# Low parts written over the exponents, head copies ahead of a high part, and the first chunk prepared a pair sooner, in an attention and two-MLP kernel

## The chip, the cores and the metric

The kernel runs on one core of a Trainium2 chip. The metric is the device time of one execution in microseconds (us), as the median of several runs. The engines of a core work side by side, each through its own list of instructions: TensorE (matmuls), ScalarE (ACT), VectorE (DVE), the Pool engine (GpSimd, POOL) and SyncE (SP), whose list here is nearly all DMA issues. They wait for each other by semaphores.

## What is computed

Attention over 4 x 8 heads, then two MLPs, all fp32:

```python
scores = scale * np.matmul(q, k.transpose(0, 1, 3, 2))      # 32 heads, 576 x 576, head_dim 64
thresh = np.max(scores, axis=-1, keepdims=True) - tau
scores = np.where(scores >= thresh, scores, -1000000000.0)
attn = softmax(scores)
x = (attn @ v) laid out as [2304, 512]
x = ((x @ w_a) * (x @ w_b)) @ w_out                          # d_ff 1536
h = x @ w_in                                                 # d_ff 1024
out = (layer_norm(h * softmax(h)) * g_ln) @ w_out2
```

## The kernel before

Each fp32 operand of a matmul is split into a high part, rounded by a copy into `fp32r`, and a low part, the difference of the two. A product is then three matmuls (high x high, high x low, low x high). The attention product of q and k packs parts so that two matmuls do. TensorE's list is written out by hand and so is that of every other engine.

**Pairs and slots.** The 32 heads go through in 16 pairs. A pair has 9 slots (`SLOTS`), one for each tile of 128 keys: head 0 of the pair has tiles 0 to 3 and half of tile 4, head 1 the other half of tile 4 and tiles 5 to 8. `MID` is 4. In slot s of a pair TensorE does, in this order (L1132 to L1143):
- `scores(s)` of the *next* pair, 4 matmuls (8 in slot 4), for the row maxima alone. It needs the maximum before it (`max_done`), since all use one PSUM place;
- `scores_t(s)` of this pair, 4 matmuls (8 in slot 4), the transposed scores. It needs `mask(s - 2)`, whose PSUM place it takes;
- `values`, the P·V matmuls at L1104. Head 0's first ones stand in slot 3, its last in slot 7; head 1's first ones in slot 8, its last in slot 2 of the next pair. The first ones of a head wait until the head before is copied out of PSUM (`head_out`).

A tile's way from `scores_t(s)` is: ScalarE `exps(s)` (L600) writes exponents to `prob`; VectorE `mask(s)` (L840) zeroes those under the threshold, reading PSUM and `prob`; ScalarE `high_probs(s)` (L607) makes `p_hi`; the Pool engine's `low_probs(s)` (L529) makes `p_lo = prob - p_hi`; TensorE reads both. `prob` has 3 places (`RAW`), `p_hi` and `p_lo` 6 each (`RP`). `exps` waits until the `p_lo` three tiles back is made.

In a slot ScalarE does, in order: `high_max` (slots 0 and 5), `exps(s)`, `high_probs(s - 1)`, then `high_v` (slots 0, 5) or `high_qk` (slots 1, 6). `copy_head` (L614) stands ahead of `exps` in slots 3 and 8. VectorE does the maximum of `scores(s)` (L826), `mask(s - 1)`, then `turn_max` (L834, slots 0 and 5), `low_qk` (L817, slots 2 and 7), `invert` (slot 6). The Pool engine does `low_max` (L537, slots 0 and 5), `split_v` (slots 1, 6), `low_probs(s - 1)`. `turn_max` needs `low_max`, `low_max` needs `high_max`. In an engine's list nothing overtakes.

SyncE deals the operands of the heads ahead: `deal_first` (zeros and high parts), `deal_low`, and the maxima by way of DRAM (`store_max`, `load_max`); it also moves finished heads to `xT` (`move_head`), spreads the row sums and stores their inverses.

**The first MLP** starts in the last pair. Its tokens go in 6 chunks of 384. Chunk 0 is prepared early: `load_inverse` (L387) brings the inverse row sums to `inverse_first`, `normalize` (L852) multiplies `xT` by them in 4 pieces, `high_x` (L634) and `low_x` (L864) split the pieces, `high_w` (L628) and `low_w` (L858) the first weights, which `load_w` (L454) brings. TensorE's `up(0, 0)` has 8 pieces; it does four of them in slots 5 to 8 of the last pair and the others between the last P·V parts. In the kernel before, `load_inverse` stands ahead of SyncE's list for pair 14, all four `normalize` pieces stand in slot 8 of pair 14, and the splits in slots 0 to 6 of pair 15. Pairs are counted from 0.

Of the kernel before, what the change touches and what calls it, by code (L numbers as in the profile page):

```python
# [23 lines left out]
P = 128  # L24
# [11 lines left out]
def build_program(nc, qkT, v_tiles, tau, w_a, w_b, w_o, w_in, w_out, g_col, eye, out):  # L36
# [20 lines left out]
    ROLL = 4  # L57
# [7 lines left out]
    RAW = 3  # L65
    RP = 6
    assert SLOTS % RAW == 0 and 2 * SLOTS % RP == 0
# [4 lines left out]
    with outer:  # L72
# [16 lines left out]
        with ExitStack() as a:  # L89
# [16 lines left out]
            prob = sb(a, "prob", [P, RAW, S])  # L106
            p_hi = sb(a, "p_hi", [P, RP, S], F32R)
            p_lo = sb(a, "p_lo", [P, RP, S], F32R)
# [200 lines left out]
        def _(sp):  # L309
# [91 lines left out]
            def step(i, e):  # L401
# [4 lines left out]
                head(load_max, i, e, 1)  # L406
                head(load_qk, i, e + 3, 0)
# [9 lines left out]
                head(load_max, i, e + 1, 0)  # L417
                pair(store_inverse, i, e - 1)
# [40 lines left out]

            for r in range(2):  # L460
                sp.wait_ge(inverse_out[r], 16 * (LAST_PAIR_OF_CHUNK_0 // 2 + (1 if r == 0 else 0)))
            load_inverse(0, inverse_first)
            step(last, 0)
            load_w(0)
# [35 lines left out]
        def _(pool):  # L500
# [23 lines left out]
            def low_probs(i, e, s):  # L524
# [3 lines left out]
                at_least(pool, pv_done, used_up(i, e, s, RP))  # L528
                pool.tensor_tensor(p_lo[:, r, :], prob[:, s % RAW, :], p_hi[:, r, :].bitcast(F32),  # L529
# [52 lines left out]
        def _(act):  # L582
# [13 lines left out]
            def exps(i, e, s):  # L596
                n, ps = number(i, e, s), st_ps[(SLOTS * e + s) % 2]
                act.wait_ge(st_done, n + 1)
                at_least(act, p_lo_done, n + 1 - RAW)
                act.activation(halves(prob[:, s % RAW, :]), ps[:, :, 0:HALF], ACT.Exp,  # L600
                               scale=SCALE).then_inc(exp_done, 1)

            def high_probs(i, e, s):
# [3 lines left out]
                act.activation(p_hi[:, r, :], prob[:, s % RAW, :], ACT.Copy).then_inc(p_hi_done, 1)  # L607
# [28 lines left out]
            def early(s):  # L636
                if s < NK:
                    if s == 0:
                        act.wait_ge(ops_in[ROLL - 1], dealt(last, ROLL - 1))
                    high_x(0, (s,))  # L640
                elif s < NK + 2:
                    high_w(0, (s - NK,))

            def step(i, e):
                for s in range(SLOTS):
                    ni, ne = pair_at(i, e + 1)
                    if s == 3 and not (isinstance(i, int) and 2 * i + e == 0):
                        pi, pe = pair_at(i, e - 1)
                        copy_head(pi, 2 * pe + 1)
# [4 lines left out]
                    if s == SLOTS - 1:  # L654
                        copy_head(i, 2 * e)
                    exps(i, e, s)
# [13 lines left out]
                    if isinstance(i, int) and 2 * i + e == PAIRS - 1:  # L670
                        early(s)
# [136 lines left out]
        def _(dve):  # L808
# [27 lines left out]
            def mask(i, e, s):  # L836
                n, ps = number(i, e, s), st_ps[(SLOTS * e + s) % 2]
                dve.wait_ge(exp_done, n + 1)
                p = halves(prob[:, s % RAW, :])
# [27 lines left out]
            def step(i, e):  # L867
                for s in range(SLOTS):
# [459 lines left out]
```

## Time and profile before

| | |
|---|---|
| median of 3 runs | 1017.98 us (1016.18 to 1018.18) |
| the profiled execution | 1015.74 us, its span 1013.60 us |
| TensorE busy | 975.0 us (96%) |
| VectorE, ScalarE, Pool engine busy | 536.9, 415.4, 256.3 us |
| TensorE granted clock | 1.00 |
| attention | about 0 to 345 us |

The span is the time from the first to the last instruction. TensorE is busy nearly everywhere; the Pool engine works only in the attention part, where VectorE is busy for about 79% of the time. Matmuls overlap by their pipelines: one of 288 columns is shown as 0.29 us, but the next starts 0.13 us after it.

### The profile page before, as it was taken

Reading aid. Unit: us, or ns where it says so; the run is one execution under the profiler, and the core shown is the slowest. Engines: PE = TensorE matmul, PEld = TensorE weight load, DVE = VectorE, ACT = ScalarE, POOL = GpSimd, SP = SyncE. Lnnn points to the kernel's source line nnn. Section 1 sums busy time; section 2 is a strip of 40 time slices with the busy share of each in tenths; the row PEclk is TensorE's granted clock in tenths of the full one; section 3 lists DMA queues with packets and bytes.
Section 4 is the critical chain, followed back from the end, with each engine's and each line's share of the span. In section 5 each row is a group of like instructions: output and inputs, shape, how many; then the busy total and the mean of one; then the engine's idle time right before and its main releaser. Section 6 shows DMA issues by size and latency. Waiting matters only on the chain.

```text
span 1013.6 us, 16645 instructions
## 1 busy us (share of the span) xinstructions
PE 975.0 (96%) x5844; PEld 924.3 (91%) x5844; DVE 536.9 (53%) x863; ACT 415.4 (41%) x739; POOL 256.3 (25%) x242
## 2 busy tenths in 40 slices
PE   5999999999998999999999999999999999999997
PEld 4999999999997999999999999999999878888886
DVE  7787878777877654321321321221223676655664
ACT  3677767777776644211211211211212422223321
POOL 3777777777777400000000000000000000000000
PEclk9999999999999999999999999999999999999999
DMA  7566666666663343210010010000020200000000
GB/s 184 148 157 156 147 152 156 161 148 150 150 151 85 108 144 108 62 32 1 1 31 0 0 31 0 0 0 0 0 83 1 82 21 21 21 21 23 28 21 31
DMA packets 51566, 71.31 MB, mean 70 GB/s; under 512 B 14552, under 2 KB 24920, under 8 KB 51536
## 3 DMA queue, kind: packets, MB, share of 16 engines
q1 hardware_dynamic: 51536, 70.94, 27.0%
q8 instruction: 16, 0.26, 0.1%
q14 instruction: 14, 0.11, 0.0%
HBM read 33.25 MB, written 5.32 MB: 38 GB/s over the span
## 4 chain that ended last, share of the span: by engine, by line
PE 91%; issue 4%; DMA 1%; SPq 1%; DVE 1%; ACT 1%; POOL 0%; POOLq 0%; DVEq 0%; ACTq 0%
PE PS L1104 12%; PE PS L1121 10%; PE PS L1123 10%; PE PS L1122 10%; PE PS L1067 8%; PE PS L1069 8%; PE PS L1191 5%; PE PS L1189 5%; PE PS L1190 5%; PE PS L1248 3%; PE PS L1250 3%; PE PS L1249 3%; PE PS L1224 3%; PE PS L1222 3%; PE PS L1223 3%
## 5 line engine op out<-in xcount | busy, mean ns | idle before, releaser
L529 POOL TENSOR_TENSOR p_lo<-prob,p_hi 128x576 fp32r<-128x576 f32 x144 | 210.1, 1460 | 80.4 <-ACT p_hi L607 79.2
L1067 PE MATMUL PS<-ops 128*128 128x288 f32 x642 | 179.2, 301 | 15.9 <-DVE ops L902 6.8
L1121 PE MATMUL PS<-x_hi,w_ab_rolled 128*128 128x384 f32 x576 | 192.5, 334 | 1.6 <-issue 1.6
L1123 PE MATMUL PS<-x_hi,w_ab_rolled 128*128 128x384 f32 x576 | 192.4, 334 | 0.0
L1122 PE MATMUL PS<-x_lo,w_ab_rolled 128*128 128x384 f32 x576 | 192.4, 334 | 0.0
L1069 PE MATMUL PS<-ops 128*128 128x288 f32 x642 | 176.2, 296 | 0.0
L941 DVE TENSOR_TENSOR gate<-gate,PS 128x384 f32<-128x384 f32 x72 | 39.9, 554 | 253.5 <-ACT gate L707 253.5
L707 ACT ACTIVATE gate<-PS 128x384 f32<-128x384 f32 x72 | 35.4, 492 | 268.7 <-PE PS L1123 268.7
L1067 PEld LDWEIGHTS PS<-ops 128*128 128x128 f32 x642 | 121.4, 189 | 21.0 <-issue 8.1
L826 DVE TENSOR_REDUCE neg_max<-PS 128x1 f32<-128x576 f32 x144 | 107.6, 749 | 47.4 <-PE PS L1069 46.4
L1069 PEld LDWEIGHTS PS<-ops 128*128 128x128 f32 x642 | 121.6, 189 | 0.0
L607 ACT ACTIVATE p_hi<-prob 128x576 fp32r<-128x576 f32 x144 | 98.6, 684 | 51.1 <-DVE prob L840 42.2
L840 DVE SCALAR_TENSOR_TENSOR prob<-PS,neg_tau,prob 128x576 f32<-128x576 f32 x144 | 116.2, 807 | 2.7 <-ACT prob L600 2.7
L568 POOL MEMSET halfpow<- 128x1 f32 x1 | 0.1, 104 | 448.0 <-PE PS L1191 448.0
L1121 PEld LDWEIGHTS PS<-x_hi,w_ab_rolled 128*128 128x128 f32 x576 | 108.2, 188 | 1.8 <-issue 1.8
L1122 PEld LDWEIGHTS PS<-x_lo,w_ab_rolled 128*128 128x128 f32 x576 | 108.1, 188 | 0.0
L1123 PEld LDWEIGHTS PS<-x_hi,w_ab_rolled 128*128 128x128 f32 x576 | 108.1, 188 | 0.0
L600 ACT ACTIVATE prob<-PS 128x576 f32<-128x576 f32 x144 | 92.9, 645 | 35.5 <-PE PS L1069 30.9
L1189 PE MATMUL PS<-g_hi,w_od 128*128 128x384 f32 x288 | 96.2, 334 | 0.0
L1190 PE MATMUL PS<-g_lo,w_od 128*128 128x384 f32 x288 | 96.2, 334 | 0.0
L1191 PE MATMUL PS<-g_hi,w_od 128*128 128x384 f32 x288 | 96.2, 334 | 0.0
L1104 PE MATMUL PS<-p_hi,v_hi 128*65 128x288 f32 x320 | 68.8, 296 | 13.7 <-issue 13.6
(91 smaller groups left out, 1530.5 us busy)
## 6 DMA issues: line engine op xcount, KB each, us to landing
qk_raw<-qkT_dram SPq DMA_DIRECT2D x32, 288.0 KB, 3.1
ops<-qk_hi SPq DMA_DIRECT2D x62, 144.0 KB
ops<-qk_hi SPq DMA_DIRECT2D x31, 288.0 KB
ops<-qk_lo SPq DMA_DIRECT2D x62, 144.0 KB
v_raw<-v_tiles_dram SPq DMA_DIRECT2D x32, 160.0 KB, 2.5
xT<-head_sb SPq DMA_DIRECT2D x32, 144.0 KB, 3.2
out_dram<-o_sb SPq DMA_DIRECT2D x18, 256.0 KB, 2.0
stage<-inverse_dram SPq DMA_DIRECT2D x20, 192.0 KB, 3.9
```

Source lines behind the costliest of these rows:

```text
L529: pool.tensor_tensor(p_lo[:, r, :], prob[:, s % RAW, :], p_hi[:, r, :].bitcast(F32), ALU.subtract).then_inc(p_lo_done, 1)
L826: dve.tensor_reduce(out=neg_max[:, e, s:s + 1], in_=ps[:, :, 0:HALF], axis=AX_XY, op=ALU.max, negate=True).then_inc(max_done, 1)
L840: dve.scalar_tensor_tensor(out=p, in0=ps[:, :, 0:HALF], scalar=neg_tau[:, 0:1], in1=p, op0=ALU.is_ge, op1=ALU.mult).then_inc(mask_done, 1)
L1067: pe.matmul(ps[:, b, 0:HALF], weights[0][:, r, own], moving[0][:, r, cols], start=(n == 0), stop=False)
L1069: ins = pe.matmul(ps[:, b, 0:HALF], weights[1][:, r, own], moving[1][:, r, cols], start=False, stop=(n == len(parts) - 1))
L1104: ins = pe.matmul(o_ps[0:D + 1, b, 0:HALF], v[:, side, t, :], p[:, r, b * HALF:(b + 1) * HALF], start=(t == 0 and part == 0), stop=(t == N ...
L1121: pe.matmul(bank, w[:, 0, :], x_hi[:, k, :], start=(k == 0), stop=False)
L1122: pe.matmul(bank, w[:, 0, :], x_lo[:, k, :], start=False, stop=False)
L1123: ins = pe.matmul(bank, w[:, 1, :], x_hi[:, k, :], start=False, stop=(k == NK - 1))
L1189: pe.matmul(bank, w[:, 0, :], g_hi[:, f % 2, :], start=(f == 0), stop=False)
L1190: pe.matmul(bank, w[:, 0, :], g_lo[:, f % 2, :], start=False, stop=False)
L1191: ins = pe.matmul(bank, w[:, 1, :], g_hi[:, f % 2, :], start=False, stop=(f == NF - 1))
```

## The change

- `p_lo` gets 9 places and `prob` the same 9 places in the same memory; the Pool engine writes `p_lo(s)` over `prob(s)`. `exps` waits for the P·V that last read the place, one pair back; `low_probs` waits for no P·V.
- `copy_head` moves from ahead of `exps` in slots 3 and 8 to behind `exps` in slots 2 and 7, ahead of a `high_probs`.
- SyncE issues `load_inverse` within its list for pair 14, behind the operands of head 31, and `load_w(0)` a few steps sooner.
- `normalize` goes one piece at a time into slots 5 to 8 of pair 14, `high_x` into slots 6 to 8 of pair 14 and slot 0 of pair 15, `high_w` into slots 1 and 2, `low_x` into slots 0 to 2, `low_w` into slots 3 and 4 of pair 15.
- TensorE's `up(0, 0)` starts in slot 4 of pair 15.

```diff
-    RAW = 3
...
-            prob = sb(a, "prob", [P, RAW, S])
+            with ExitStack() as same:
+                prob = sb(same, "prob", [P, SLOTS, S])
+            p_lo = sb(a, "p_lo", [P, SLOTS, S], F32R)
             p_hi = sb(a, "p_hi", [P, RP, S], F32R)
-            p_lo = sb(a, "p_lo", [P, RP, S], F32R)
...
                 head(load_max, i, e, 1)
+                if isinstance(i, int) and 2 * i + e == PAIRS - 2:
+                    for r in range(2):
+                        sp.wait_ge(inverse_out[r], 16 * (LAST_PAIR_OF_CHUNK_0 // 2 + (1 if r == 0 else 0)))
+                    load_inverse(0, inverse_first)
                 head(load_qk, i, e + 3, 0)
...
                 head(load_max, i, e + 1, 0)
+                if isinstance(i, int) and 2 * i + e == PAIRS - 2:
+                    load_w(0)
                 pair(store_inverse, i, e - 1)
...
             step(last - 1, 1)
-            for r in range(2):
-                sp.wait_ge(inverse_out[r], 16 * (LAST_PAIR_OF_CHUNK_0 // 2 + (1 if r == 0 else 0)))
-            load_inverse(0, inverse_first)
             step(last, 0)
-            load_w(0)
             step(last, 1)
...
                 pool.wait_ge(p_hi_done, n + 1)
-                at_least(pool, pv_done, used_up(i, e, s, RP))
-                pool.tensor_tensor(p_lo[:, r, :], prob[:, s % RAW, :], p_hi[:, r, :].bitcast(F32),
+                pool.tensor_tensor(p_lo[:, s, :], prob[:, s, :], p_hi[:, r, :].bitcast(F32),
...
                 act.wait_ge(st_done, n + 1)
-                at_least(act, p_lo_done, n + 1 - RAW)
+                at_least(act, pv_done, used_up(i, e, s, SLOTS))
...
-            def early(s):
-                if s < NK:
-                    if s == 0:
-                        act.wait_ge(ops_in[ROLL - 1], dealt(last, ROLL - 1))
-                    high_x(0, (s,))
-                elif s < NK + 2:
-                    high_w(0, (s - NK,))
+            def early(pair, s):
+                if pair == PAIRS - 2 and s == SLOTS - NK + 1:
+                    for r in (2, 3):
+                        act.wait_ge(ops_in[r], dealt(last, r))
+                k = SLOTS * (pair - PAIRS + 2) + s - (SLOTS - NK + 1)
+                if 0 <= k < NK:
+                    high_x(0, (k,))
+                elif NK <= k < NK + 2:
+                    high_w(0, (k - NK,))
...
-                    if s == 3 and not (isinstance(i, int) and 2 * i + e == 0):
-                        pi, pe = pair_at(i, e - 1)
-                        copy_head(pi, 2 * pe + 1)
...
-                    if s == SLOTS - 1:
+                    exps(i, e, s)
+                    if s == 2 and not (isinstance(i, int) and 2 * i + e == 0):
+                        pi, pe = pair_at(i, e - 1)
+                        copy_head(pi, 2 * pe + 1)
+                    if s == SLOTS - 2:
                         copy_head(i, 2 * e)
-                    exps(i, e, s)
                     if s > 0:
                         high_probs(i, e, s - 1)
...
-                    if isinstance(i, int) and (2 * i + e, s) == (PAIRS - 2, SLOTS - 1):
-                        for r in range(ROLL):
-                            dve.wait_ge(head_moved[r], 16 * (heads // ROLL - 1))
-                        normalize(0, inverse_first)
+                    if isinstance(i, int) and 2 * i + e == PAIRS - 2 and s >= SLOTS - NK:
+                        if s == SLOTS - NK:
+                            for r in range(2):
+                                dve.wait_ge(head_moved[r], 16 * (heads // ROLL - 1))
+                        normalize(0, inverse_first, (s - (SLOTS - NK),))
                     if isinstance(i, int) and 2 * i + e == PAIRS - 1:
-                        if 1 <= s <= NK:
-                            low_x(0, (s - 1,))
-                        if NK < s <= NK + 2:
-                            low_w(0, (s - NK - 1,))
+                        low_x(0, ((0,), (1, 2), (3,))[s] if s < 3 else ())
+                        if s in (3, 4):
+                            low_w(0, (s - 3,))
...
-                    if final and s >= 5:
-                        if s == 5:
+                    if final and s >= 4:
+                        if s == 4:
                             pe.wait_ge(max_done, SLOTS * PAIRS)
-                        up(0, 0, True, range(s - 5, s - 4))
+                        up(0, 0, True, ((0,), (1, 2), (3,), (4,), (5,))[s - 4])
...
             values(last, 1, 1, *prev[0])
-            up(0, 0, True, range(4, 5))
+            up(0, 0, True, (6,))
             values(last, 1, 1, *prev[1])
-            up(0, 0, True, range(5, 6))
+            up(0, 0, True, (7,))
             values(last, 1, 1, *prev[2])
-            up(0, 0, True, range(6, 2 * NK))
```

## Rows read from the trace of the kernel before

**Rows 1.** Stage windows: us, then busy us of PE, PEld, DVE, ACT, POOL.

```profile
31.36:290.30 258.94, 247.71 (x1822) 240.53 (x1821) 205.28 (x299) 191.44 (x339) 194.26 (x169) 1.00 0.64 152
```

**Rows 2.** TensorE's waits over the span: total us, times, longest.

```profile
PE PS L1104 <- issue: 13.6, 30, 1.0
```

**Rows 3.** Timeline of TensorE, pairs 8 and 9: start, us, line, operands, count.

```profile
195.06 0.43 PE L1104 MATMUL PS<-p_lo,v_hi 128*65 128x288 f32 x2
...
196.25 0.29 PE L1069 MATMUL PS<-ops 128*128 128x288 f32 x1
197.03 0.44 PE L1104 MATMUL PS<-p_hi,v_hi 128*65 128x288 f32 x2 [0.50 <-issue]
...
198.37 0.29 PE L1067 MATMUL PS<-ops 128*128 128x288 f32 x1
...
203.92 0.42 PE L1104 MATMUL PS<-p_lo,v_hi 128*65 128x288 f32 x2
...
205.12 0.29 PE L1069 MATMUL PS<-ops 128*128 128x288 f32 x1
205.82 0.45 PE L1104 MATMUL PS<-p_hi,v_hi 128*65 128x288 f32 x2 [0.41 <-issue]
...
206.90 0.29 PE L1067 MATMUL PS<-ops 128*128 128x288 f32 x1
```

**Rows 4.** Timeline of ScalarE in the same pairs: `exps` and head copies.

```profile
195.04 0.63 ACT L600 ACTIVATE prob<-PS 128x576 f32<-128x576 f32 x1
...
196.22 0.72 ACT L614 ACTIVATE head_sb<-PS,guard 65x576 f32<-65x576 f32 x1
...
203.61 0.63 ACT L600 ACTIVATE prob<-PS 128x576 f32<-128x576 f32 x1
...
205.00 0.72 ACT L614 ACTIVATE head_sb<-PS,guard 65x576 f32<-65x576 f32 x1
```

**Rows 5.** Timeline of VectorE in the same pairs.

```profile
195.43 1.34 DVE L817 TENSOR_TENSOR qk_lo<-qk_raw,qk_hi 128x576 fp32r<-128x576 f32 x1
...
196.69 0.74 DVE L826 TENSOR_REDUCE neg_max<-PS 128x1 f32<-128x576 f32 x1
197.36 0.80 DVE L840 SCALAR_TENSOR_TENSOR prob<-PS,neg_tau,prob 128x576 f32<-128x576 f32 x1
...
201.52 0.81 DVE L840 SCALAR_TENSOR_TENSOR prob<-PS,neg_tau,prob 128x576 f32<-128x576 f32 x1
...
204.21 1.12 DVE L817 TENSOR_TENSOR qk_lo<-qk_raw,qk_hi 128x576 fp32r<-128x576 f32 x1
205.26 0.75 DVE L826 TENSOR_REDUCE neg_max<-PS 128x1 f32<-128x576 f32 x1
```

**Rows 6.** Timeline of the Pool engine in the same pairs.

```profile
194.72 1.44 POOL L529 TENSOR_TENSOR p_lo<-prob,p_hi 128x576 fp32r<-128x576 f32 x1
...
199.12 1.44 POOL L529 TENSOR_TENSOR p_lo<-prob,p_hi 128x576 fp32r<-128x576 f32 x1 [1.07 <-ACT p_hi L607]
200.51 0.21 POOL L537 TENSOR_TENSOR max_cols<-neg_max,max_cols 128x5 fp32r<-128x5 f32 x1
...
203.29 1.44 POOL L529 TENSOR_TENSOR p_lo<-prob,p_hi 128x576 fp32r<-128x576 f32 x1
```

**Rows 7.** Timeline of TensorE in the last two pairs: starts after a wait.

```profile
307.89 0.37 PE L1067 MATMUL PS<-ops 128*128 128x288 f32 x1 [1.14 <-DMA ops<-qk_lo]
...
322.57 0.40 PE L1067 MATMUL PS<-ops 128*128 128x288 f32 x1 [2.04 <-DVE prob L840]
...
327.78 0.45 PE L1104 MATMUL PS<-p_hi,v_hi 128*65 128x288 f32 x2 [1.04 <-issue]
...
333.47 0.41 PE L1121 MATMUL PS<-x_hi,w_ab_rolled 128*128 128x384 f32 x1 [1.56 <-issue]
```

**Rows 8.** Timeline of SyncE's issues: the four loads of `load_inverse`.

```profile
297.32 2.67 SPq L387 DMA_DIRECT2D inverse_first<-inverse_dram  x4
```

**Rows 9.** Timeline of VectorE: the four pieces of `normalize`.

```profile
318.39 3.40 DVE L852 TENSOR_TENSOR xT<-xT,inverse_first 128x384 f32<-128x384 f32 x4
```

More of the change, by code:

```diff
@@ L64, in build_program @@
     LOW = 16
-    RAW = 3
     RP = 6
-    assert SLOTS % RAW == 0 and 2 * SLOTS % RP == 0
+    assert 2 * SLOTS % RP == 0
     assert D == 64 and REST == 64 and FK == NK * P and heads % ROLL == 0
@@ L598, in exps @@
                 act.wait_ge(st_done, n + 1)
-                at_least(act, p_lo_done, n + 1 - RAW)
-                act.activation(halves(prob[:, s % RAW, :]), ps[:, :, 0:HALF], ACT.Exp,
+                at_least(act, pv_done, used_up(i, e, s, SLOTS))
+                act.activation(halves(prob[:, s, :]), ps[:, :, 0:HALF], ACT.Exp,
                                scale=SCALE).then_inc(exp_done, 1)
@@ L606, in high_probs @@
                 at_least(act, pv_done, used_up(i, e, s, RP))
-                act.activation(p_hi[:, r, :], prob[:, s % RAW, :], ACT.Copy).then_inc(p_hi_done, 1)
+                act.activation(p_hi[:, r, :], prob[:, s, :], ACT.Copy).then_inc(p_hi_done, 1)
             def copy_head(i, j):
@@ L669, in step @@
                         high_qk(mi, 2 * me + 1)
-                    if isinstance(i, int) and 2 * i + e == PAIRS - 1:
-                        early(s)
+                    if isinstance(i, int):
+                        early(2 * i + e, s)
             high_qk(0, 0)
@@ L838, in mask @@
                 dve.wait_ge(exp_done, n + 1)
-                p = halves(prob[:, s % RAW, :])
+                p = halves(prob[:, s, :])
                 dve.scalar_tensor_tensor(out=p, in0=ps[:, :, 0:HALF], scalar=neg_tau[:, 0:1], in1=p,
@@ L846, in invert, with normalize @@
                 dve.reciprocal(inverse[:, e, :], sum_spread[:, e, :]).then_inc(inverse_done, 1)
-            def normalize(c, place):
+            def normalize(c, place, ks=range(NK)):
                 dve.wait_ge(inverse_in, INVERSE_LOADS * (c + 1))
-                for k in range(NK):
+                for k in ks:
                     x = xT[:, k, bass.ds(c * CH, CH)]
@@ L1101, in values @@
                         pe.wait_ge(p_hi_done, n + 1)
-                    v, p = v_lo if part == 1 else v_hi, p_lo if part == 2 else p_hi
+                    v = v_lo if part == 1 else v_hi
+                    p = p_lo[:, s, :] if part == 2 else p_hi[:, r, :]
                     for b in range(2):
-                        ins = pe.matmul(o_ps[0:D + 1, b, 0:HALF], v[:, side, t, :], p[:, r, b * HALF:(b + 1) * HALF],
+                        ins = pe.matmul(o_ps[0:D + 1, b, 0:HALF], v[:, side, t, :], p[:, b * HALF:(b + 1) * HALF],
                                         start=(t == 0 and part == 0), stop=(t == NT - 1 and part == 2))
```

## The prediction, made blind

> **What bounds the kernel now.** I read the stage windows first. Over 13 pairs of heads TensorE is busy for 247.71 of 258.94 us, and no other engine passes 80% [rows 1], so one pair takes 258.94 / 13 = 19.92 us and TensorE sets the pace, except for its own gaps. After 345 us nothing is touched by the change, so all that can move lies in the pairs and in the last two of them.
>
> Next the waits of TensorE: 13.6 us in 30 idle stretches ahead of line 1104, the P·V matmuls [rows 2]. The reader is to see on TensorE's timeline where they are [rows 3]. Matmuls of 288 columns start 0.13 us apart. Two places in a pair break that step. In slot 8, P·V starts at 197.03 after a matmul started at 196.25: 0.78 where 0.13 would do, 0.65 lost. In slot 3 it is 205.82 after 205.12: 0.57 lost. Both starts follow the end of ScalarE's copy of the finished head: 196.22 + 0.72 = 196.94 and 205.00 + 0.72 = 205.72 [rows 4], each 0.09 to 0.10 before TensorE goes on. That 0.09 is what I take as the price of one hand-over between engines.
>
> So the head copy is late. It isn't waiting for TensorE: the last P·V of the head ends at 195.06 + 0.43 = 195.49 and at 203.92 + 0.42 = 204.34 [rows 3]. It stands in ScalarE's order behind one `high_probs`.
>
> **The copy moved ahead, slot 3.** The new place is behind `exps(2)`, which ends at 203.61 + 0.63 = 204.24 [rows 4]; P·V ends at 204.34. The copy can run from 204.42 to 205.14 and TensorE sees it at 205.23. TensorE is free at 205.12 + 0.13 = 205.25 [rows 3]. All 0.57 us are gained. `high_probs(1)` now comes one copy (0.72) later and ends where the copy ended before, near 205.75; its first reader is the fourth P·V group of slot 3, six matmuls (0.8 us) behind 205.25, so 0.3 of cover is left.
>
> **The copy moved ahead, slot 8.** The new place is behind `exps(7)`, which ends at 195.04 + 0.63 = 195.67 [rows 4]. The copy ends at 196.39, TensorE sees it at 196.48 and is free at 196.38 [rows 3]. The copy's wait shrinks by 0.55. But what is late next? `scores_t(0)` of the next pair, at 198.37 [rows 3], needs `mask(7)`, since that frees its PSUM half. `mask(7)` ends at 197.36 + 0.80 = 198.16 [rows 5], and it isn't waiting for TensorE or for the copy. VectorE is busy without a break in `low_qk` (195.43 to 196.77), `max(8)` (196.69 to 197.43), `mask(7)`. And `low_qk` itself ends when it does because of the Pool engine: `p_lo(5)` ends at 194.72 + 1.44 = 196.16, `low_qk` 0.61 later; in slot 3 `p_lo(0)` ends at 203.29 + 1.44 = 204.73, `low_qk` at 204.21 + 1.12 = 205.33, 0.60 later [rows 5, 6]. So TensorE may start `scores_t(0)` at 198.16 + 0.09 = 198.25 and not sooner. The gain of slot 8 is 198.37 - 198.25 = 0.12 us of 0.65; the rest turns into a wait ahead of line 1067 (`max(8)` ends at 197.43 and is needed by `scores(0)`, then `mask(7)`).
>
> The Trainium skill (SBUF — State Buffer, SBUF: two separate sides) says that a VectorE operation with two SBUF inputs and a GpSimd operation exclude each other for a whole instruction, not that they share. By that rule, the two rows agreeing, `low_qk` ends at a fixed distance behind `p_lo(5)`, and the later `p_lo(6)` changes nothing. If they shared instead, it would come out as the second case below.
>
> **Does the gain last?** I follow the same chain on. `mask(7)` (198.16), `high_probs(7)`, `p_lo(7)` (199.12 to 200.56), `low_max` (from 200.51), `turn_max`, `max(1)`, `mask(0)` (201.52 to 202.33), `high_probs(0)`, `p_lo(0)` (to 204.73), `low_qk` (to 205.33), `max(3)` (205.26 + 0.75 = 206.01) [rows 5, 6]: none of these waits for TensorE, so none moves. TensorE needs `max(3)` for `scores(4)`, which starts at 206.90 [rows 3]; with both gains it wants to start at 206.90 - 0.57 - 0.12 = 206.21, and may from 206.01 + 0.09 = 206.10. That is 0.11 to spare. From `scores(4)` on everything hangs on TensorE and moves with it. So a pair gains 0.57 + 0.12 = **0.69 us**, and could gain 0.80 at most before this chain binds: the new pair is 19.23.
>
> **Nine places.** `exps` no longer waits for `p_lo` three tiles back but for P·V nine tiles back. `exps(3)`, behind the copy that ends at 205.72, needed `p_lo(0)`, which had ended at 204.73 [rows 4, 6], so the old wait was already free there; the new one looks back a whole pair. Both at nothing; were it not for the nine places, the later `high_probs` would eat into that distance. The subtraction on the Pool engine now writes over its own operand. No row shows that on the Pool engine. Above nothing I can't bound it by a row of the same engine; on VectorE the mask already writes over `prob` in 0.81 us [rows 5]. I take 0, and price it as a rival.
>
> **The sum over the pairs.** Pairs 1 to 13: 13 x 0.69 = 9.0. Pair 0 has slot 8 alone, 0.1. Pair 14 has slot 3, about 0.5. Together 9.6 us.
>
> **The last two pairs.** Four things:
> - The four loads of `load_inverse` take SyncE from 297.32 to 299.99, ahead of the operands of head 31; TensorE then starts `scores(4)` at 307.89 after 1.14 idle [rows 7, 8], 1.31 against a 0.13 step with what the pipeline hides. Moved behind those operands they hold nobody that TensorE needs; what they are now ahead of (`load_v`, the moving of heads) is used a slot or more later. The 1.3 is gained.
> - The four normalizes, 3.40 us in one block, end in TensorE's wait of 2.04 [rows 7, 9]. They go one by one into slots 5 to 8 of pair 14, where VectorE has 1.34 less to do in slot 7 (no `low_qk`). Added there are 3.40 - 1.34 = 2.1 us that TensorE sees through `mask(5)` to `mask(7)`. One wait for another of the same size: 0. If the first meets a `p_lo` it costs up to 1.44 more, if none does 1 less.
> - The high parts of the chunk are gone from pair 15's slots 1 to 3: the copy there, with its 1.04 idle, comes sooner. Of the 1.04 I count a third, since `low_x` now stands ahead of `mask(0)` and `mask(1)`.
> - `up` waits 1.56 at 333.47 for the first low weights, which now come two slots sooner [rows 7]. That should go, but VectorE, the Pool engine and ScalarE carry the same work, and the waits for masks grow. Of the 1.56 I count a third.
>
> Together 1.3 + 0 + 0.35 + 0.5 = **2.2 us**, with ends at -0.5 (the normalizes meet `p_lo`) and 1.3 + 1.04 + 1.56 = 3.9.
>
> **Sum.** 9.6 + 2.2 = 11.8 us. Against the span of 1013.60 that is 1001.8; the profiled execution took 1015.74, so 1003.9; the median of the runs is 2.24 above it, 1017.98 - 11.8 = **1006.2 us**.
>
> **The rivals and their chances.** About 0.2% (2 us) is what a measurement of this kernel can tell from no change.
> 1. As forecast, 1006.2: 0.50.
> 2. VectorE and the Pool engine share instead of excluding. `low_qk` of slot 7 overlapped `p_lo(6)` by the last 0.3 us; with `p_lo(6)` a copy later it would end some 0.16 sooner and `mask(7)` with it: 14 x 0.16 = 2.2 more, 1004.0. Against it stand the equal 0.60 and 0.61. 0.10.
> 3. TensorE sets the whole pace: the chain of VectorE loosens once ScalarE is earlier. 13 x (0.57 + 0.65) + 0.65 + 0.5 = 17.0, and the end's 3.9: 997.1. Against it: `mask(7)` doesn't wait for ScalarE. 0.12.
> 4. Slot 8 gives nothing and neither does the end: 13 x 0.57 + 0.5 = 7.9, 1010.1; with the end at -0.5, 1010.6. For it: two engines' orders are tight in pair 14. 0.18.
> 5. The change doesn't do what it says: the copy is held by `exps` or P·V as long as before. Then only the load's 1.3 remains, 1016.7. P·V's end at 204.34 and 195.49 speaks against it. 0.04.
> 6. Slower. Writing over its own operand takes the Pool engine d longer. `p_lo(3)`, `p_lo(5)`, `p_lo(7)` and `p_lo(0)` all lie on the chain above (the first through `low_max` of slot 5), so a pair loses 4d beyond the 0.11 to spare. It decides from d = (11.8 / 14 + 0.11) / 4 = 0.24 us, that is 1.68 in place of 1.44. At d = 0.4 the time is 1006.2 + 14 x (1.6 - 0.11) = 1027. 0.06.
>
> Faster holds cases 1 to 4, 0.90; within 0.2% case 5, 0.04; slower case 6, 0.06. The range reaches from just above case 3 to beyond case 4: 998 to 1012. That leaves out 3, 5 and 6 in the main, 0.2.
>
> **What would show it.** In the changed kernel: the pair's period 19.2 us; idle ahead of line 1104 nearly gone, a wait ahead of the first or the fifth matmul of slot 0 for `max(8)` or `mask(7)` of about half a us in its place; `p_lo` still 1.44 us; `low_qk` still ending 0.6 us after a `p_lo`; no DMA wait in pair 14; masks as releasers in pairs 14 and 15. A period of 18.8 would make my chain wrong; one of 19.4 the slot 3 term; `p_lo` above 1.5 us the whole sum.

## The result and the profile after

| | before | changed |
|---|---|---|
| median | 1018.08 us (4 runs, 1016.18 to 1018.52) | 1003.23 us (4 runs, 1002.93 to 1004.75) |
| ratio | | 0.9861, 95% interval 0.9844 to 0.9878 |
| profiled execution, its span | 1015.74, 1013.60 us | 1002.93, 1001.10 us |
| TensorE busy | 975.0 us (96%) | 978.4 us (98%) |

The changed kernel is 1.4% faster. The forecast was 1006.2 us in a range of 998 to 1012.

The medians differ by 14.9 us, the profiled executions by 12.8: that of the kernel before lies 2.3 us under its median, that of the changed kernel 0.3 under. What follows compares the profiled ones; the other 2 us come back under "Why the prediction was right".

TensorE's waits in the changed kernel come first (total us, times, longest). Of the 13.6 us ahead of the P·V matmuls [rows 2], 0.3 are left. Line 1104 is now 1112, and 1067 is 1074.

```profile
PE PS L1074 <- DVE neg_max L833: 3.6, 5, 1.1
...
PE PS L1074 <- DVE prob L847: 1.8, 2, 1.5
...
PE PS L1112 <- issue: 0.3, 1, 0.3
```

To see where the time went, I cut both spans at four marks: the first matmul of `scores(4)` in pair 1 (mark 1), in pair 13 and in pair 14, and the first matmul of the second product (`down`). The marks of the changed kernel on TensorE's timeline:

```profile
47.92 0.29 PE L1074 MATMUL PS<-ops 128*128 128x288 f32 x1
...
278.21 0.29 PE L1074 MATMUL PS<-ops 128*128 128x288 f32 x1
...
297.42 0.29 PE L1074 MATMUL PS<-ops 128*128 128x288 f32 x1
...
336.88 0.33 PE L1196 MATMUL PS<-g_hi,w_od 128*128 128x384 f32 x1
```

The kernel before has them at 47.55, 286.70, 307.89 [rows 7] and 349.39.

| stretch | before | changed | gain |
|---|---|---|---|
| start to mark 1 | 47.55 | 47.92 | -0.37 |
| 12 pairs | 239.15 (19.93 each) | 230.29 (19.19 each) | 8.86 |
| pair 13 to 14 | 21.19 | 19.21 | 1.98 |
| to the first `down` | 41.50 | 39.46 | 2.04 |
| the rest | 664.21 | 664.22 | -0.01 |

These sum to the 12.5 us by which the spans differ. The forecast was 11.8.

Next, the place that the forecast had called the new bound, slots 7 and 8 and the next slot 0. TensorE (start, us, line, operands, count):

```profile
191.67 0.46 PE L1112 MATMUL PS<-p_hi,v_hi 128*65 128x288 f32 x2
...
192.24 0.43 PE L1112 MATMUL PS<-p_lo,v_hi 128*65 128x288 f32 x2
192.71 0.39 PE L1074 MATMUL PS<-ops 128*128 128x288 f32 x1
192.94 0.30 PE L1076 MATMUL PS<-ops 128*128 128x288 f32 x1
...
193.36 0.40 PE L1074 MATMUL PS<-ops 128*128 128x288 f32 x1
193.59 0.29 PE L1076 MATMUL PS<-ops 128*128 128x288 f32 x1
```

ScalarE, VectorE and the Pool engine there:

```profile
189.09 0.69 ACT L610 ACTIVATE p_hi<-prob 128x576 fp32r<-128x576 f32 x1 [0.43 <-DVE prob L847]
...
190.26 0.63 ACT L603 ACTIVATE prob<-PS 128x576 f32<-128x576 f32 x1
190.83 0.74 ACT L617 ACTIVATE head_sb<-PS,guard 65x576 f32<-65x576 f32 x1
```

```profile
190.73 1.19 DVE L824 TENSOR_TENSOR qk_lo<-qk_raw,qk_hi 128x576 fp32r<-128x576 f32 x1
191.83 0.75 DVE L833 TENSOR_REDUCE neg_max<-PS 128x1 f32<-128x576 f32 x1
192.50 0.80 DVE L847 SCALAR_TENSOR_TENSOR prob<-PS,neg_tau,prob 128x576 f32<-128x576 f32 x1
```

```profile
187.70 1.42 POOL L532 TENSOR_TENSOR p_lo<-prob,p_hi 128x576 fp32r<-128x576 f32 x1 [0.26 <-ACT p_hi L610]
189.08 0.81 POOL L525 TENSOR_TENSOR v_lo<-v_raw,v_hi 128x320 fp32r<-128x320 f32 x1
189.86 1.44 POOL L532 TENSOR_TENSOR p_lo<-prob,p_hi 128x576 fp32r<-128x576 f32 x1
```

The copy now ends at 191.57 and P·V starts at 191.67. `max(8)` ends at 192.58, and `scores(0)` starts at 192.71, 0.47 behind the last pair of P·V matmuls where 0.27 would do. `mask(7)` ends at 193.30, and `scores_t(0)` starts at 193.36. So the wait did pass from the copy to `max(8)` and `mask(7)`, and `low_qk` still ends 0.62 behind `p_lo(5)` (191.92 against 191.30), as in [rows 5, 6]. The hand-over is 0.06 here, not 0.09. Each of the two stops also costs something behind it: the next matmul starts 0.23 later (192.94 and 193.59) and not 0.13, so 0.10 each.

### The profile page after: what moved, and what is told of

Its sections match the earlier page's. It is cut to its first block, busy times and chain, and to the rows that moved or that the text cites. A ratio compares the mean times of both kernels' runs of the same rounds, so it can differ in the third digit from the quotient of the medians.

```text
span 1001.1 us, 16500 instructions
## 1 busy us (share of the span) xinstructions
PE 978.4 (98%) x5844; PEld 926.6 (93%) x5844; DVE 530.6 (53%) x863; ACT 414.8 (41%) x739; POOL 253.3 (25%) x242
## 4 chain that ended last, share of the span: by engine, by line
PE 90%; issue 3%; DVE 3%; DMA 1%; ACT 1%; POOL 1%; SPq 1%; DVEq 0%; POOLq 0%; ACTq 0%
PE PS L1112 11%; PE PS L1129 10%; PE PS L1130 10%; PE PS L1131 10%; PE PS L1074 8%; PE PS L1076 7%; PE PS L1197 5%; PE PS L1196 5%; PE PS L1198 5%; PE PS L1255 3%; PE PS L1257 3%; PE PS L1256 3%; PE PS L1231 3%; PE PS L1229 3%; PE PS L1230 3%
## 5 line engine op out<-in xcount | busy, mean ns | idle before, releaser
L532 POOL TENSOR_TENSOR p_lo<-prob,p_hi 128x576 fp32r<-128x576 f32 x144 | 208.1, 1447 | 71.7 <-ACT p_hi L610 69.5
L1074 PE MATMUL PS<-ops 128*128 128x288 f32 x642 | 183.8, 308 | 14.8 <-DVE ops L909 6.6
L1076 PE MATMUL PS<-ops 128*128 128x288 f32 x642 | 178.1, 298 | 0.0
L1074 PEld LDWEIGHTS PS<-ops 128*128 128x128 f32 x642 | 122.6, 191 | 25.0 <-issue 12.2
L1076 PEld LDWEIGHTS PS<-ops 128*128 128x128 f32 x642 | 123.0, 192 | 0.0
```

What stands on the lines that cost most here:

```text
L532: pool.tensor_tensor(p_lo[:, s, :], prob[:, s, :], p_hi[:, r, :].bitcast(F32), ALU.subtract).then_inc(p_lo_done, 1)
L1074: pe.matmul(ps[:, b, 0:HALF], weights[0][:, r, own], moving[0][:, r, cols], start=(n == 0), stop=False)
L1076: ins = pe.matmul(ps[:, b, 0:HALF], weights[1][:, r, own], moving[1][:, r, cols], start=False, stop=(n == len(parts) - 1))
```

## Experiments

Below, "period" is the time from mark 1 to the mark of pair 13 divided by 12. All come from TensorE's timeline of one execution of each kernel. Kernels whose pairs are alike agree to 0.2 us over the 12 pairs (239.15 in the kernel before and in chunk_only; 230.29, 230.31 and 230.15 in the changed kernel, copy_places and xlo_later), so a profile alone tells 0.02 us per pair. A time without a median is that of one execution. The edits are shown in short form.

### The copies alone

```diff
 # kernel before
-                    if s == 3 and not first_pair: copy_head(pi, 2 * pe + 1)
-                    if s == SLOTS - 1: copy_head(i, 2 * e)
                     exps(i, e, s)
+                    if s == 2 and not first_pair: copy_head(pi, 2 * pe + 1)
+                    if s == SLOTS - 2: copy_head(i, 2 * e)
```

> The kernel before with the head copies moved and nothing else (three places of prob, separate p_lo, chunk 0 prepared late). Theory A (the copy is the whole gain of the loop, the nine places are worth nothing): the period of a pair is 19.19 us as in the changed kernel (13 periods, 249.5), so 9.4 us less over the loop, 0.7 in pair 13 to 14 and some 0.7 in pair 15: about 10.8 us below the kernel before, ratio 0.989. Rival B (the nine places are needed, since exps waits for a p_lo three tiles back which the later high parts delay): waits of exps for p_lo appear on ScalarE and the period stays at 19.5 or more, 5 us or less gained, ratio 0.995 or higher.

Measured: 1009.47 us median of 5, ratio 0.9917 (0.9904 to 0.9930).

The marks are at 47.78 and 279.88. Period 232.10 / 12 = 19.34. That lies between the theories: the copies give 0.59 of the 0.74 us per pair. ScalarE's waits show none for a `p_lo`, so rival B's mechanism isn't there either; something else of the nine places is worth 0.15 per pair. TensorE stops in slot 0 as in the changed kernel, and longer.

### The nine places alone

```diff
 # kernel before
-            prob = sb(a, "prob", [P, RAW, S]); p_lo = sb(a, "p_lo", [P, RP, S], F32R)
+            prob and p_lo: [P, SLOTS, S] in the same memory
-                at_least(act, p_lo_done, n + 1 - RAW)
+                at_least(act, pv_done, used_up(i, e, s, SLOTS))
-                at_least(pool, pv_done, used_up(i, e, s, RP))
```

> The kernel before with p_lo written over prob, nine places for both, and nothing else. Theory A: period 19.92, p_lo 1.44 us as before, time the same within 1 us, ratio 1.000. Rival B (the places alone loosen ScalarE): 1 to 3 us faster. Rival C (the Pool engine is slower over its own operand): p_lo above 1.5 us and the period up by four times the difference; slower.

Measured: 1016.45 us median of 12 against 1017.96 of 20, ratio 0.9987 (0.9976 to 0.9997).

The marks are at 48.46 and 287.62: period 19.93, as before. In the loop the places alone are worth nothing. Writing over its own operand costs the Pool engine nothing either: `p_lo` takes 1447 ns on average against 1460 before. So the 0.13% of the ratio has no place in the loop. Some 0.3 us of it lie outside the span: the time is longer than the span by 1.8 us here and by 2.1 in the kernel before. The interval allows 0.3 to 2.4 us, so whether there is more is open.

### The copies with the nine places

> The kernel before with the copies moved and the nine places, chunk 0 prepared late as before. Theory A: the period is the changed kernel's, 19.19; the last two pairs are as long as with the copies alone (scores(4) of pair 14 at 20.7 behind that of pair 13, 42.7 us from there to the first matmul of the second product), so near 1007. Rival B (the last two pairs gain from the places): 41.5 or less there.

Both edits above together. Measured: 1007.34 us in one execution.

The marks are at 47.91, 278.22 and, in pair 14:

```profile
298.76 0.37 PE L1067 MATMUL PS<-ops 128*128 128x288 f32 x1 [1.14 <-DMA ops<-qk_lo]
```

Period 19.19, the changed kernel's. The places are worth 0.15 per pair once the copies are out of the way. The DMA wait ahead of `scores(4)` of pair 14 is there as before, 20.54 behind pair 13. From there to the first `down` (at 341.32) it is 42.56 us: theory A.

### The wait that went with the places

What did the nine places take away? A second wait of the Pool engine ahead of `p_lo`. Look at how far `p_lo(3)` starts behind the end of its `p_hi`, in the run with the copies alone and in the changed kernel:

```profile
185.94 0.68 ACT L607 ACTIVATE p_hi<-prob 128x576 fp32r<-128x576 f32 x1
...
186.78 1.43 POOL L529 TENSOR_TENSOR p_lo<-prob,p_hi 128x576 fp32r<-128x576 f32 x1 [0.86 <-ACT p_hi L607]
```

```profile
185.09 0.68 ACT L610 ACTIVATE p_hi<-prob 128x576 fp32r<-128x576 f32 x1
...
185.85 1.44 POOL L532 TENSOR_TENSOR p_lo<-prob,p_hi 128x576 fp32r<-128x576 f32 x1 [0.96 <-ACT p_hi L610]
```

It is 0.16 against 0.08. So I put the wait back into the changed kernel, nothing else:

```diff
 # changed kernel
                 pool.wait_ge(p_hi_done, n + 1)
+                at_least(pool, pv_done, used_up(i, e, s, RP))
```

> The changed kernel with one wait more ahead of each p_lo on the Pool engine, the one for the P·V of six tiles back that the change took out; it is long satisfied. In the traces with it p_lo starts 0.15 us behind the end of p_hi, without it 0.07. Theory A (a satisfied second wait costs 0.08 on the Pool engine, and four p_lo lie on the chain of a pair): the period rises from 19.19 to 19.34 as in the run with the copies alone, 2 us more in all, near 1005. Rival B (the 0.15 us between the run with the copies alone and the changed kernel comes from the three places of prob): the period stays at 19.19.

The marks are at 47.13 and 279.24: period 232.11 / 12 = 19.34, time 1004.43. Theory A: the satisfied wait makes up the whole difference between 19.34 and 19.19.

But not every satisfied second wait has this price. The Pool engine's list has a loop for pairs 2 to 13; pairs 0, 1, 14 and 15 are written out one by one. Here is the run with the wait put back, first in the loop, then behind it:

```profile
187.15 0.69 ACT L611 ACTIVATE p_hi<-prob 128x576 fp32r<-128x576 f32 x1 [0.41 <-PE PS L1113]
...
310.25 0.69 ACT L611 ACTIVATE p_hi<-prob 128x576 fp32r<-128x576 f32 x1 [0.22 <-DVE prob L848]
```

```profile
188.00 1.44 POOL L533 TENSOR_TENSOR p_lo<-prob,p_hi 128x576 fp32r<-128x576 f32 x1 [0.27 <-ACT p_hi L611]
...
311.01 1.44 POOL L533 TENSOR_TENSOR p_lo<-prob,p_hi 128x576 fp32r<-128x576 f32 x1 [0.44 <-ACT p_hi L611]
```

The gap is 0.16 in the loop and 0.07 behind it, with the same two waits. It is so in all four kernels that have the second wait: of the 102 to 106 `p_lo` seen in each one's loop none starts less than 0.15 behind its `p_hi`, and of the 30 to 39 outside most start at 0.07 or 0.08 (only the first six of a kernel have no second wait). In the three without it the least gap in the loop is 0.07. So the price belongs to this wait as it stands in the loop. What makes it there no run shows.

### The Pool engine's share of the pace

First p_lo made shorter, then longer.

```diff
 # changed kernel, half_low
-                pool.tensor_tensor(p_lo[:, s, :], prob[:, s, :], p_hi[:, r, :].bitcast(F32),
+                pool.tensor_tensor(p_lo[:, s, 0:HALF], prob[:, s, 0:HALF], p_hi[:, r, 0:HALF].bitcast(F32),
...
-                        p[:, b * HALF:(b + 1) * HALF]
+                        p[:, 0:HALF] if part == 2 else p[:, b * HALF:(b + 1) * HALF]
```

> The changed kernel with the Pool engine making only the first 288 columns of each p_lo; TensorE reads those columns twice for the low part, so the low parts of the other half are left out of the result, and TensorE does as many matmuls of the same size. Theory A (p_lo(3), p_lo(5), p_lo(7), p_lo(0) lie on the chain that paces a pair): with p_lo at about 0.75 the low_qk of slot 7 ends some 0.7 sooner, the waits in slot 0 of a pair go, and the period falls to TensorE's own 18.7 to 18.8: 5 us below the changed kernel, near 996 to 998. Rival B (VectorE's own work in slots 7 and 8 paces, whatever the Pool engine does): the period stays at 19.1 to 19.2, within 1 us of the changed kernel.

```profile
L532 POOL TENSOR_TENSOR p_lo<-prob,p_hi 128x288 fp32r<-128x288 f32 x144 | 116.6, 810 | 152.6 <-ACT p_hi L610 152.6
```

The marks are at 47.74 and 273.35. With `p_lo` at 0.81 us the period is 225.61 / 12 = 18.80 and the time 994.79: theory A. TensorE then loses less than 0.2 us of a pair to stops, so 18.80 is nearly what it needs by itself, and the changed kernel's pair loses 0.39 to the Pool engine's subtraction. Rival B falls.

```diff
 # changed kernel, long_low
+                at_least(pool, pad_done, n)
+                pool.tensor_tensor(pool_pad[:, :], p_hi[:, r, 0:64].bitcast(F32), p_hi[:, r, 0:64].bitcast(F32),
+                                   ALU.subtract).then_inc(pad_done, 1)
                 pool.tensor_tensor(p_lo[:, s, :], prob[:, s, :], p_hi[:, r, :].bitcast(F32),
```

> The changed kernel with a small subtraction of 64 columns into a scrap tile on the Pool engine ahead of each p_lo, with one wait more. It makes each p_lo d longer, d between 0.25 and 0.35 us by the row of low_max (0.21) and the price of a wait. Theory A (four p_lo on the chain that paces a pair): the period rises by 4d, 1.0 to 1.4 us, to 20.2 to 20.6; near 1018 to 1023. Rival B (two p_lo at most): by 0.5 to 0.7, to 19.8.

The marks are at 47.99 and 287.66: period 239.67 / 12 = 19.97, time 1014.61. How long is d? `p_hi`, the scrap subtraction and `p_lo` of one tile:

```profile
179.39 0.69 ACT L615 ACTIVATE p_hi<-prob 128x576 fp32r<-128x576 f32 x1 [1.03 <-DVE prob L852]
```

```profile
180.16 0.29 POOL L535 TENSOR_TENSOR pool_pad<-p_hi 128x64 f32<-128x64 f32 x1 [0.59 <-ACT p_hi L615]
180.41 1.44 POOL L537 TENSOR_TENSOR p_lo<-prob,p_hi 128x576 fp32r<-128x576 f32 x1
```

The scrap subtraction starts 0.08 behind the end of `p_hi`, as `p_lo` does in the changed kernel, though it has a second wait, and in the loop. `p_lo` starts 0.25 behind that. So d is 0.25. The period rose by 0.78, that is 3.1 d; with the extra wait alone it was 0.15 for d = 0.08, 1.9 d. Rival B allows 0.5 for this d, and 0.78 is beyond it; theory A asks 1.0, and 0.78 falls short.

Where the time goes shows more than the two ratios. In nine pairs in the middle, counted from `scores(4)`, `p_lo(5)` ends at 9.05 to 9.08 in the changed kernel, at 9.20 to 9.22 with the extra wait and at 9.61 to 9.67 here; `mask(7)` ends 2.0 behind it in all three. So the extra wait's 0.15 comes up by `p_lo(5)`, and so do 0.58 of the 0.78. The other 0.20 come in slots 2 to 4, where TensorE now stops ahead of `scores_t(2)` and, shortly, of `scores(4)`:

```profile
178.69 0.40 PE L1079 MATMUL PS<-ops 128*128 128x288 f32 x1 [0.37 <-DVE neg_max L838]
...
183.57 0.29 PE L1081 MATMUL PS<-ops 128*128 128x288 f32 x1
183.79 0.40 PE L1079 MATMUL PS<-ops 128*128 128x288 f32 x1
```

The first of these is `scores(0)`, the last the fifth matmul of slot 2, 0.22 behind the one before it. That stop lies behind `low_max` and `turn_max` of slot 0, and thus behind `p_lo(7)`. With a small d two `p_lo` count, with a larger one those of the other half of the pair as well.

### Which of them: low_max taken out, low_qk moved

```diff
 # changed kernel, max_early: on ScalarE high_max, on the Pool engine low_max
-                    if s == 0: high_max / low_max (i, 2 * e + 1)
-                    if s == MID + 1: high_max / low_max (ni, 2 * ne)
+                    if s == MID: high_max / low_max (ni, 2 * ne)            # before high_probs(s - 1), low_probs(s - 1)
+                    if s == SLOTS - 1: high_max / low_max (ni, 2 * ne + 1)
```

> The changed kernel with high_max and low_max one step earlier (in slots 4 and 8, right behind exps and ahead of the high part and the p_lo of the tile before), turn_max where it was. Theory A (the pace of a pair is set by a chain of VectorE, ScalarE and Pool that passes p_lo(3) and p_lo(7) only because low_max stands behind them): VectorE's wait of 0.65 to 0.8 ahead of turn_max goes, the waits of TensorE in slot 0 go too, the period falls from 19.19 to 18.8, about 5 us over the loop and some more in the last two pairs: near 997, ratio to the first kernel 0.979. Rival B (the chain mask(5), p_lo(5), low_qk, max(8), mask(7) alone still paces): the period stays above 19.1, within 1 us of the changed kernel's 1003.2.

Measured: 1000.77 us median of 5, ratio 0.9834 (0.9821 to 0.9848).

The marks are at 48.06 and 278.05. VectorE's wait ahead of `turn_max` is gone, but the period is 229.99 / 12 = 19.17, only 0.02 lower: rival B. TensorE's wait in slot 0 stays where it was:

```profile
192.63 0.40 PE L1078 MATMUL PS<-ops 128*128 128x288 f32 x1 [0.20 <-DVE neg_max L837]
```

So the path through `low_max` isn't the only one that sets the pace. In the changed kernel (ScalarE's and the Pool engine's rows above) `p_lo(5)` is held from two sides at once. `p_hi(5)` ends at 189.78, 0.08 ahead of it, which is the usual gap; its `mask(5)` stands behind `turn_max`, `low_max` and `p_lo(3)`. And `p_lo(4)`, `split_v` and `p_lo(5)` run from 187.70 to 191.30 without a gap. In max_early the first side is off and the second holds:

```profile
188.90 0.69 ACT L612 ACTIVATE p_hi<-prob 128x576 fp32r<-128x576 f32 x1 [0.33 <-DVE prob L851]
```

```profile
189.01 0.82 POOL L525 TENSOR_TENSOR v_lo<-v_raw,v_hi 128x320 fp32r<-128x320 f32 x1
189.78 1.44 POOL L532 TENSOR_TENSOR p_lo<-prob,p_hi 128x576 fp32r<-128x576 f32 x1
```

`p_lo(5)` starts 0.19 behind `p_hi(5)` and right behind `split_v`, at the same time in the pair as before. Either side has two `p_lo` in it, `p_lo(3)` and `p_lo(5)` or `p_lo(4)` and `p_lo(5)`, which fits the 1.9 d. Nobody moved `split_v`, so what the second side is worth alone is not shown.

The kernel gains 1.2 us in the last two pairs (from 297.26 to 335.50, 38.24 against 39.46). By the medians max_early is the fastest kernel of the study that computes everything, 2.5 us below the changed kernel; the two intervals overlap, so that it beats the changed kernel isn't settled.

```diff
 # changed kernel, lowqk8
-                    if s == 7 and exists(mi, me):
+                    if s == 8 and exists(mi, me):
                         low_qk(mi, 2 * me + 1)
```

> The changed kernel with low_qk of a pair's second head in slot 8 behind mask(7), not in slot 7 ahead of max(8). Theory A (what paces a pair is the path mask(4), p_lo(4), split_v, p_lo(5), low_qk, max(8), mask(7), scores_t(0), in which low_qk can't end before p_lo(5) does): max(8) and mask(7) come 0.5 us or more sooner, the 0.4 us lost in slot 0 go, and the period falls from 19.19 to between 18.85 and 18.95, where TensorE alone needs 18.80: near 999. Rival B (the later low_qk holds max(0), mask(8) and turn_max of the next pair by as much): the wait moves to slot 1 and the period stays at 19.1 or more.

Measured: 1016.11 us in one execution, a period of 20.26, a miss for both theories: rival B's "19.1 or more" allows it, but its wait in slot 1 isn't the one that came. The new wait is a DMA's:

```profile
190.31 0.37 PE L1074 MATMUL PS<-ops 128*128 128x288 f32 x1 [0.96 <-DMA ops<-qk_lo]
```

SyncE's issues and VectorE's `low_qk` in the pair behind show why:

```profile
199.14 0.38 SPq L380 DMA_DIRECT2D inverse_dram<-inverse  x1
202.60 0.34 SPq L315 DMA_DIRECT2D qk_raw<-qkT_dram  x1
```

```profile
200.84 1.59 DVE L824 TENSOR_TENSOR qk_lo<-qk_raw,qk_hi 128x576 fp32r<-128x576 f32 x1
```

`load_qk` waits for `low_qk`, and behind `load_qk` in SyncE's list stand the move of the head and the dealing of the next operands. SyncE stood still from 199.52 to 202.60. Thus the run doesn't tell whether VectorE's path would have loosened; that the path by `p_lo(5)` and `low_qk` paces rests on half_low, on the two longer `p_lo` and on the rows, not on this.

### One copy alone

```diff
 # changed kernel
-                    if s == SLOTS - 2: copy_head(i, 2 * e)   # behind exps(7)
+                    if s == SLOTS - 1: copy_head(i, 2 * e)   # ahead of exps(8)
```

> The changed kernel with the copy of slot 8 put back to where it was, ahead of exps(8), so that only the copy of slot 3 is moved. Theory A (slot 3 gives its 0.57 whole, slot 8 gives only what mask(7) leaves, 0.12 to 0.23 of 0.65): the period is 19.31 to 19.42; an idle stretch ahead of the P·V of slot 8 comes back; near 1005. Rival B (both copies give alike): 19.55 or more, near 1008.

The marks are at 47.12 and 279.73. Period 232.61 / 12 = 19.38, time 1005.07: theory A. Against 19.93, slot 3 gives 0.55; from 19.38 to 19.19, slot 8 gives 0.19 of the 0.65 that TensorE had lost there. Both kernels have the nine places. With the Pool engine's second wait in place the two copies give 0.59 together, so if slot 3 gives 0.55 there too, slot 8 gives only 0.04: 0.15 of its 0.19 need the wait gone.

### The last two pairs

```diff
 # kernel before, chunk_only: all of the change on chunk 0 (load_inverse, load_w(0), normalize,
 # high_x, high_w, low_x, low_w, up), nothing on the copies and the places
```

> The kernel before with chunk 0 prepared a pair sooner and nothing else (load_inverse behind the operands of head 31, normalize, high and low parts and the first weights moved, up starting in slot 4). Theory A: the loop is unchanged at 19.92; the DMA wait of 1.3 us ahead of scores(4) of pair 14 goes, and the rest of the last two pairs gives 1.3 to 2: about 3 us below the kernel before, ratio 0.997. Rival B (the end needs the earlier copies too): only the 1.3, ratio 0.9985.

Measured: 1014.83 us median of 8, ratio 0.9977 (0.9965 to 0.9988).

```profile
287.63 0.29 PE L1072 MATMUL PS<-ops 128*128 128x288 f32 x1
...
307.52 0.29 PE L1072 MATMUL PS<-ops 128*128 128x288 f32 x1
...
348.11 0.44 PE L1193 MATMUL PS<-g_hi,w_od 128*128 128x384 f32 x1 [0.17 <-DVE g_lo L948]
```

No DMA wait ahead of `scores(4)`: 19.89 in place of 21.19, so 1.3 gained. Behind it 40.59 in place of 41.50, 0.9 gained. Together 2.2, a little under the "about 3" of theory A and above rival B's 1.3.

What is left there in the changed kernel is one wait of 1.48 ahead of `scores_t(2)` of the last pair:

```profile
314.07 0.40 PE L1074 MATMUL PS<-ops 128*128 128x288 f32 x1 [1.48 <-DVE prob L847]
```

```profile
311.61 1.68 DVE L871 TENSOR_TENSOR x_lo<-xT,x_hi 128x384 fp32r<-128x384 f32 x1
313.22 0.80 DVE L847 SCALAR_TENSOR_TENSOR prob<-PS,neg_tau,prob 128x576 f32<-128x576 f32 x1
```

```profile
311.46 1.42 POOL L532 TENSOR_TENSOR p_lo<-prob,p_hi 128x576 fp32r<-128x576 f32 x1
```

The `low_x` started 0.15 us behind a `p_lo`, ended 0.41 behind its end, and took 1.68 us where the one at 325.82 in the kernel before took 0.55; `mask(0)` came behind it. I moved it:

```diff
 # changed kernel, xlo_later
-                        low_x(0, ((0,), (1, 2), (3,))[s] if s < 3 else ())
+                        low_x(0, ((), (0, 1), (2, 3))[s] if s < 3 else ())
```

> The changed kernel with low_x moved one slot back in the last pair (pieces 0 and 1 behind mask(0), 2 and 3 behind mask(1)), so that nothing of chunk 0 stands between turn_max and mask(0). Theory A (the largest wait left at the end, 1.5 us ahead of scores_t(2), comes from a low_x that the Pool engine's p_lo keeps off for 1.7 us): that wait goes, some of it comes back ahead of scores_t(3); from scores(4) of pair 14 to the first matmul of the second product 38.3 to 38.9 in place of 39.46 us, the loop unchanged: near 1002. Rival B (the work is only moved): 39.3 or more.

```profile
298.56 0.29 PE L1074 MATMUL PS<-ops 128*128 128x288 f32 x1
...
316.33 0.40 PE L1074 MATMUL PS<-ops 128*128 128x288 f32 x1 [0.93 <-DVE prob L847]
...
319.81 0.37 PE L1074 MATMUL PS<-ops 128*128 128x288 f32 x1 [1.62 <-DVE prob L847]
...
338.70 0.33 PE L1196 MATMUL PS<-g_hi,w_od 128*128 128x384 f32 x1
```

It is 40.14 us in place of 39.46, worse by 0.7: the wait split in two and grew. Rival B, and beyond it.

### All three moves

The edits of max_early, lowqk8 and xlo_later in one kernel.

> The changed kernel with all three: high_max and low_max one step earlier, low_qk of the second head behind mask(7), low_x a slot later. Theory A (with the path by p_lo(5) gone, the one by low_max is the next that binds, and it is gone too): a period of 18.80 to 18.85, TensorE's own, and the end of xlo_later: near 996, ratio to the first kernel 0.978 to 0.980. Rival B (one of the moves undoes another): no faster than the kernel with high_max and low_max early, 1000.8.

Measured: 1015.16 us median of 7, ratio 0.9972 (0.9961 to 0.9984). The DMA waits of lowqk8 are all there. Rival B: one move undoes the rest.

## Why the prediction was right, and where it wasn't

**Slot 3**: right. 0.57 forecast, 0.55 measured.

**Slot 8**: the mechanism was right and the size off. I said that the copy's wait would pass to `mask(7)`, 0.12 gained of 0.65. Changed kernel against slot3_only it was 0.19, but by the sums above only 0.04 with the second wait in place. One term is missing in my sum: a stop costs 0.10 more behind it, and TensorE now stops ahead of `scores_t(0)` (193.36, then 193.59), where it didn't. Against that the hand-over that I priced at 0.09 is 0.06 for this pair of engines. 0.12 - 0.10 + 0.03 is 0.05. With the wait gone `p_lo(5)` starts 0.80 behind the end of `mask(5)` instead of 0.88, and `mask(7)` ends 0.15 sooner.

**Nine places, at nothing**: wrong. The step looked at what the old waits waited *for* and found them satisfied. It left out that a wait can cost something when it is satisfied. The second wait on the Pool engine cost 0.08 us per `p_lo` in the loop, 0.15 us per pair, 2 us in all. It stayed invisible as long as the copy's stall was there to cover it, which is why the places alone changed nothing in the loop.

**Does the gain last**: the answer was right, and the chain in the main too. Its price was 4d beyond 0.11 to spare, that is 0.21 for d = 0.08 and 0.89 for d = 0.25; measured were 0.15 and 0.78. So the four `p_lo` cost a little less than I said. I left out that `p_lo(4)` and `split_v` hold `p_lo(5)` just as late as the chain does, and I let every d count, while TensorE sets the pace of slots 1 to 5 nearly by itself as long as d is small. By an estimate the break-even of the slower rival would have been near d = 0.3 and not 0.24: at 0.25 the run is still 2.9 us below the kernel before (1017.46, the median taken alongside), and from d = 0.08 to 0.25 the time rose by 10.2 us.

Slots 3 and 8 with the places give 0.74 per pair where 0.69 was forecast; 12 pairs make up 0.6 us of the difference.

**The load behind the operands**: right, 1.3 us, in the changed kernel and in the chunk's run alike.

**The end**: too low. Forecast behind `scores(4)` of pair 14 was 0.85, measured 2.04. The waits there, before against after (idle and restart together, from the steps of TensorE's timeline): the normalizes 2.3 against 1.8; the copy of slot 3, 1.2 against 0.4; the first weights 1.8 against none, where I had counted a third; the copies of slot 8, 1.0 against none, which I had left out for these two pairs; and against these a new 1.7 ahead of `scores_t(2)` and 0.4 ahead of the second weights. I had named masks as what would be late next, and they are. Two terms were too small: the first weights, where I took a third of a wait that went whole, and the copies of slot 8, which I had left out.

**The start**: 0.7 us of the forecast gain lay ahead of mark 1 (slot 8 of pair 0 and slot 3 of pair 1), and the changed kernel's execution is 0.4 us later there. That is mostly chance: xlo_later has the same lists up to there, and its mark 1 is at 49.19, 1.3 us later still. One thing that differs is the pace of TensorE at the very start. Its matmuls of 288 columns start 0.24 us apart until 9.6 us in the kernel before and until 16 us in the changed one, then 0.13; the granted clock is shown as 1.00 in both.

**The sum**: 11.8 against 12.5 for the spans is in part luck. The start came out 1.1 us under the forecast, the end 1.2 over and the 12 pairs 0.6 over. In these pairs the wait gave 1.8 us that I had at nothing, and the copies gave less than I said.

**From the span to the median**: I carried the 2.24 us by which the median lay above the profiled execution over to the changed kernel. There it is 0.30, which is 1.9 of the 3.0 us by which the forecast was too high. The rest is 0.7 of the span and 0.3 that lie outside it: in the four kernels with the wait on the Pool engine for old P·V the profiled time is 2.10 to 2.14 longer than the span, in the ten without it 1.75 to 1.84. As to the 1.9, the mean granted clock gives a hint. Of 40 executions of the kernel before, the 9 with 1.000 took 1016.5 us on average and the 31 below it 1018.1. Of the changed kernel's four, three had 1.000. The last section shows what lowers it.

The sharing rival (0.10) is not borne out: `low_qk` ends 0.62 behind `p_lo(5)` although `p_lo(6)` now starts after it, at 192.22.

## What to carry over

When two engines' orders are moved against a wait, ask for the next late thing at the same place before counting the gain: here 0.65 us of stall gave 0.19, since the mask that is needed next was late for another reason. On a chain through the Pool engine look at the gap behind each wait in the loop itself, satisfied waits too, and take out those that another wait already implies. A path that is off in an experiment and changes nothing may still have been binding: look whether a second one ends at the same time. And before an operation is moved to a later slot, look who waits for it in SyncE's list: what is queued behind that one DMA issue moves as well.

## What the runs showed of the hardware

A satisfied semaphore wait ahead of a Pool operation can delay it by 0.08 us. In the loop, `p_lo` with two waits starts 0.15 to 0.17 behind the end of `p_hi` in four kernels, with one wait 0.07 to 0.09 in three. Outside the loop the same two waits show 0.07 to 0.08, and so, mostly, does the scrap subtraction of long_low with its two waits in the loop.

A stop of TensorE ahead of a q·k matmul costs about 0.10 us beyond the wait: the next matmul of 288 columns starts 0.23 later instead of 0.13. Ahead of P·V it is only some 0.02: the second pair starts 0.28 to 0.29 later (197.31 behind 197.03 and 206.11 behind 205.82 in the kernel before) instead of 0.26 to 0.27.

TensorE's clock can fall to half after a stall. In the kernel with the nine places alone, after TensorE had waited 2.02 us in the last pair, the windows show (stretch, busy us of PE, PEld, DVE, ACT, POOL, then the granted clock, DMA share, GB/s):

```profile
318.90:323.50 4.60, 2.57 (x18) 2.29 (x18) 4.60 (x8) 1.89 (x5) 2.88 (x3) 1.00 0.67 200
...
324.10:327.20 3.10, 3.10 (x15) 3.00 (x14) 2.39 (x4) 2.36 (x6) 2.96 (x3) 0.50 0.04 7
```

For 3.1 us, between stretches at 1.00, the granted clock is 0.50, the lower of its two levels (1.2 of 2.4 GHz), and matmuls of 288 columns start 0.24 us apart. That costs about half of the 3.1 us. The same stall of 2.04 us in the kernel before [rows 7] was followed by a clock of 1.00. The runs of the copies alone and of the copies with the places had the dip too, behind waits of 2.65 and 2.66. The changed kernel, whose longest wait there is 1.48, had none, and xlo_later with 1.62 had none. Five traces have a second dip of the same kind between 12 and 18 us; in the kernel of the places alone it comes with a wait of 1.46. None of these traces is that of the kernel before or of the changed kernel. By this a stall that is cut is worth more than its own length, now and then. The length of the wait alone doesn't sort the cases: 2.02 had a dip and 2.04 had none.
